# A fused attention and feed-forward kernel: the low parts of the hidden rows move from VectorE to GpSimd

## The reference

```python
def _moe_ref(x, w_gate, w_val, w_out, rms_g):
    rms = np.sqrt(np.mean(x * x, axis=-1, keepdims=True) + 1e-06)
    xn = x / rms * rms_g
    g = xn @ w_gate
    silu = g * (1.0 / (1.0 + np.exp(-g)))
    val = xn @ w_val
    return (silu * val @ w_out).astype(np.float32)
```

## Time and profile before

| | us |
|---|---|
| median of 3 runs | 306.15 |
| lowest, highest | 305.89, 306.91 |
| the profiled execution, its own time | 306.57 |
| its span, first to last instruction | 304.3 |
| TensorE busy in the span | 291.7 |
| VectorE busy | 223.0 |
| ScalarE busy | 165.7 |
| GpSimd busy | 29.8 |

### The profile page before, as it was taken

The page is one execution under the profiler, slowest core; times in us unless marked ns, Lnnn a source line. Parts: engine busy times, 40 slices in busy tenths (PEclk is TensorE's granted clock), DMA queues, the critical chain, the costliest instruction groups (busy, mean ns, idle before and its releaser), DMA issues.

```text
span 304.3 us, 6596 instructions
## 1 busy us (share of the span) xinstructions
PE 291.7 (96%) x2595; PEld 238.0 (78%) x2595; DVE 223.0 (73%) x428; ACT 165.7 (54%) x314; POOL 29.8 (10%) x50
## 2 busy tenths in 40 slices
PE   7789999999999999999999999999999999999983
PEld 7677788888888887888888878887888778797572
DVE  4746977976887879768877797688678767975414
ACT  2565665645656556446565564465546556557422
POOL 1266001000100010003400100020010000000000
PEclk9999999999999999999999999999999999999997
DMA  7999400000013000100130001999300100010007
GB/s 191 324 223 221 101 2 1 2 0 2 0 17 72 19 0 13 28 0 2 16 87 4 0 15 24 380 373 312 68 10 0 26 11 0 13 24 2 2 4 293
DMA packets 34928, 21.94 MB, mean 72 GB/s; under 512 B 19537, under 2 KB 31570, under 8 KB 34898
## 3 DMA queue, kind: packets, MB, share of 16 engines
q1 hardware_dynamic: 34610, 21.23, 26.0%
q10 hardware_dynamic: 288, 0.30, 0.4%
HBM read 17.45 MB, written 2.23 MB: 65 GB/s over the span
## 4 chain that ended last, share of the span: by engine, by line
PE 85%; DVE 4%; DMA 4%; SPq 2%; ACT 2%; issue 2%; DVEq 0%; ACTq 0%
PE bank L956 81%; DMA area<-in_moe_w_out 4%; PE bank L995 2%; PE bank L1029 1%; DVE hl L813 1%; SPq L341 1%; DVE area L948 1%; DVE hid L807 1%; ACT woh L594 1%; DVE area L725 0%; PE bank L1107 0%; DVE cmax_a L864 0%; DVE area L699 0%; PE bank L1042 0%; SPq L347 0%
## 5 line engine op out<-in xcount | busy, mean ns | idle before, releaser
L807 DVE TENSOR_TENSOR hid<-bank,silu 128x512 f32<-128x512 f32 (+1 forms) x108 | 71.0, 658 | 48.2 <-PE bank L956 25.9
L545 ACT ACTIVATE silu<-bank 128x512 f32<-128x512 f32 (+1 forms) x108 | 62.0, 574 | 67.2 <-PE bank L956 66.3
L813 DVE TENSOR_TENSOR hl<-hid,hh 128x512 fp32r<-128x512 f32 (+1 forms) x108 | 71.1, 658 | 0.0
L553 ACT ACTIVATE hh<-hid 128x512 fp32r<-128x512 f32 (+1 forms) x108 | 65.0, 602 | 4.3 <-DVE hid L807 4.3
L956 PE MATMUL bank<-xh,wgh 128*128 128x512 f32 (+1 forms) x108 | 42.9, 397 | 1.8 <-DVE xl L776 1.3
L956 PE MATMUL bank<-hh,woh 128*128 128x512 f32 (+1 forms) x108 | 43.5, 402 | 0.0
L956 PE MATMUL bank<-xh,wvh 128*128 128x512 f32 (+1 forms) x108 | 41.1, 380 | 0.0
L956 PE MATMUL bank<-xh,wvl 128*128 128x512 f32 (+1 forms) x108 | 41.1, 380 | 0.0
L956 PE MATMUL bank<-hh,wol 128*128 128x512 f32 (+1 forms) x108 | 41.1, 380 | 0.0
L956 PE MATMUL bank<-xh,wgl 128*128 128x512 f32 (+1 forms) x108 | 41.0, 380 | 0.0
L956 PE MATMUL bank<-hl,woh 128*128 128x512 f32 (+1 forms) x108 | 40.9, 378 | 0.0
(11 more groups left out here) (147 smaller groups left out, 345.7 us busy)
## 6 DMA issues: line engine op xcount, KB each, us to landing
area<-in_moe_w SPq DMA_DIRECT2D x1, 4096.0 KB, 13.6
area<-in_moe_w SPq DMA_DIRECT2D x8, 512.0 KB, 7.2
q_in<-in_q SPq DMA_DIRECT2D x16, 128.0 KB, 2.8
y_nat<-in_v SPq DMA_DIRECT2D x4, 512.0 KB, 7.1
out<-area SPq DMA_DIRECT2D x8, 256.0 KB, 2.2
area<-in_k SPq DMA_DIRECT2D x14, 128.0 KB, 5.9
y_nat<-area SPq DMA_DIRECT2D x112, 16.0 KB, 1.8
area<-in_moe_w_gate SPq DMA_DIRECT2D x1, 768.0 KB, 7.0
```

The source lines that it names most:

```text
L545: act.activation(silu[n][:, 0:w], gate_b[n][:, 0:w], ACT.Silu).then_inc(s_silu_ready, 1)
L553: act.activation(hh[m % NH][:, 0:w], hid[m % 2][:, 0:w], ACT.Copy).then_inc(s_hh_ready, 1)
L807: dve.tensor_tensor(hid[n][:, 0:w], val_b[n][:, 0:w], silu[n][:, 0:w], ALU.mult).then_inc(s_hid_ready, 1)
L813: dve.tensor_tensor(hl[m % NH][:, 0:w], hid[m % 2][:, 0:w], hh[m % NH][:, 0:w].bitcast(F32), ALU.subtract).then_inc(s_hl_ready, 1)
```

## The change

In `step` of VectorE the low part is left out for the chunks counted 12 to 95 over all blocks, which are all 84 chunks of blocks 1 to 7; those of block 0 and of the narrow block 8 stay. GpSimd makes them instead (`hidden_lo`), in one list with the inverse roots and the row subtractions: the low part of chunk c + 2 in iteration c, the inverse root behind that of iteration 5, the row subtraction behind that of iteration 9. As the first iterations that it covers are 10 and 11 of block 0, each block has its own twelve spread over two iterations of the block before and ten of its own. Two waits join the two engines' turns, one at each end (`s_hl_ready` at C and at C * NB). The constants for the third stage are made in block 0, ahead of the first inverse root of the loop. VectorE's maximum `cmax_a` gets a wait for the copy of the logits, `s_logit_ready`.

```diff
--- before.py
+++ after.py
@@ -320,6 +320,10 @@
 
             return j + 2 <= NB
 
+        def by_pool(i):
+
+            return C <= i < C * NB
+
         def keys_in(j):
 
             return j // 2 + 1 if j % 2 == 0 and j // 2 + 1 < B else 0
@@ -454,25 +458,38 @@
                                    r_blk[:, j, 0:nt].unsqueeze(2).to_broadcast([P, nt, NS]), ALU.subtract)\
                     .then_inc(s_cshift_ready, 1)
 
-            inverse_rms(1)
-            for j in range(2, NB):
-                inverse_rms(j)
-                combine_shift(j - 2)
-                if j == 4:
-                    pool.memset(slotZ[:, :], 0.0)
-                    pool.memset(hTz[:, :, :, :], 0.0).then_inc(done, 1)
-                    pool.memset(ones[:, :], 1.0).then_inc(done, 1)
-                    for n in range(-3, 4):
-
-                        pool.wait_ge(done, 9 + n)
-                        pool.affine_select(out=rep[:, :], in_=rep[:, :], compare_op=ALU.not_equal, fill=1.0, base=NS * n,
-                                           pattern=[[-1, P]], channel_multiplier=1).then_inc(done, 1)
-                if j == 6:
-                    pool.wait_ge(s_vaug_ready, B)
-                    pool.memset(y_nat[:, :, P], 1.0).then_inc(done, 1)
-                    pool.memset(comb[:, NT:NTP, :], 0.0).then_inc(done, 1)
-            inverse_rms(NB)
-            for j in (NB - 2, NB - 1, NB):
+
+            pool.memset(slotZ[:, :], 0.0)
+            pool.memset(hTz[:, :, :, :], 0.0).then_inc(done, 1)
+            pool.memset(ones[:, :], 1.0).then_inc(done, 1)
+            for n in range(-3, 4):
+
+                pool.wait_ge(done, 9 + n)
+                pool.affine_select(out=rep[:, :], in_=rep[:, :], compare_op=ALU.not_equal, fill=1.0, base=NS * n,
+                                   pattern=[[-1, P]], channel_multiplier=1).then_inc(done, 1)
+
+            def hidden_lo(i):
+                m = i % C
+                pool.wait_ge(s_hh_ready, i + 1)
+                pool.tensor_tensor(hl[m % NH][:, :], hid[m % 2][:, :], hh[m % NH][:, :].bitcast(F32), ALU.subtract)\
+                    .then_inc(s_hl_ready, 1)
+
+            for j in range(NB):
+                for c in range(C):
+                    i = C * j + c + LAG - 1
+                    if i == C:
+                        pool.wait_ge(s_hl_ready, C)
+                    if by_pool(i):
+                        hidden_lo(i)
+                    if c == 5:
+                        inverse_rms(j + 1)
+                    if c == 9 and j > 0:
+                        combine_shift(j - 1)
+                    if c == 10 and j == 5:
+                        pool.wait_ge(s_vaug_ready, B)
+                        pool.memset(y_nat[:, :, P], 1.0).then_inc(done, 1)
+                        pool.memset(comb[:, NT:NTP, :], 0.0).then_inc(done, 1)
+            for j in (NB - 1, NB):
                 combine_shift(j)
 
 
@@ -809,6 +826,10 @@
                 jm = j if m < C else j + 1
                 if m >= 0 and (m < C or j < NB):
                     w, i = width(jm), C * j + m
+                    if by_pool(i):
+                        return
+                    if i == C * NB:
+                        dve.wait_ge(s_hl_ready, C * NB)
                     dve.wait_ge(s_hh_ready, i + 1)
                     dve.tensor_tensor(hl[m % NH][:, 0:w], hid[m % 2][:, 0:w], hh[m % NH][:, 0:w].bitcast(F32),
                                           ALU.subtract).then_inc(s_hl_ready, 1)
@@ -861,6 +882,7 @@
                         logits(j - 1)
                     if j == NB - 1 and c == 9:
 
+                        dve.wait_ge(s_logit_ready, NB - 1)
                         dve.tensor_reduce(cmax_a[:, :], logit[:, 0:NC, :].rearrange("p t s -> p s t"), axis=AX.X, op=ALU.max)
                     if last and c == 2:
```

## The result

The changed kernel takes 307.74 us (median of 20 runs, 307.01 to 310.6), the kernel before 305.58 (median of 20, 304.8 to 307.13). The ratio is 1.007, 95% interval 1.0054 to 1.0086: slower by 2.2 us. Forecast were 308.15 us and +2.0.

What follows compares the result with a forecast made beforehand. TensorE was taken to bound the kernel, busy throughout 36 to 257 us. 306.57 + 2.3 - 0.3 = 308.6, 0.4 over the median, so 308.15 us, 0.65% slower; case range 307.3 to 309.0, 8-in-10 range 305.6 to 309.4.

Steps and rivals of the forecast that it cites:

- TensorE can't gain in blocks 1 to 6: From 36 to 257 us TensorE is busy for all of 221.00 us, so taking low parts from VectorE shortens nothing there.
- The low parts on GpSimd have room: GpSimd takes 1.28 us for each low part; late ones cost 0, covered by 1.4 us more of room.
- GpSimd first, then x_n held until it ends, plus 0.55: Blocks 1 to 6: GpSimd starts chunk 8's low part 0.10 us earlier; normalised rows x_n end 0.55 us after it.
- VectorE first: Rival: VectorE starts x_n before GpSimd's low part, so x_n is not held; 305.85 us, no change; chance 0.32.
- The mean is not held: Blocks 1 to 6: the mean square on VectorE ends at its usual length despite GpSimd's low part of chunk 7.
- the mean is held too: Rival, blocks 1 to 6: mean square waits for GpSimd's chunk 7 low part; 0.58 us a block, 309.35 us; chance 0.12.
- the term of +2.3 us: Late x_n makes TensorE lose 0.38 us in each of blocks 1 to 6: 6 x 0.38 = +2.3 us.
- 0.17 us of a late load are absorbed: TensorE weight loads: from block 0's feature transposes, 0.51 us late costs 0.34, so 0.17 is absorbed.
- VectorE is busy for 58 us less: Profile after, whole kernel: VectorE busy for about 58 us less, GpSimd for 108 us more.
- step 2 of the layout: Block 3: the low part behind chunk 8's `hid` goes, which held VectorE's queue for 0.60 us; the mean ends at 137.36.
- Block 7 loses nothing, its end gains 0.3: Block 7: half-wide x_n is ready before its load, no loss; at the end -0.3 us, ends 0 and -0.5.

Runs made afterwards that it cites:

- wait experiment: Changed kernel, but GpSimd waits for the normalised rows x_n before chunk 8's low part in blocks 1 to 7: 304.89 us, ratio 0.9976 to the kernel before.
- memset experiment: Kernel before, with two memsets of 128 x 1024 on GpSimd ahead of the inverse root in blocks 1 to 6: 306.1 us, ratio 0.9999.
- chunk 7 experiment: Changed kernel, with chunk 7's low part, ahead of the inverse root, back on VectorE: 309.4 us, ratio 1.0128 to the kernel before.
- dummy experiment: Kernel before, with an unused 128 x 512 subtraction on GpSimd right behind the inverse root in blocks 1 to 6: 310.82 us, ratio 1.0167.
- with the copy: Kernel before, with an unused 128 x 512 copy on GpSimd behind the inverse root in blocks 1 to 6: 306.94 us, ratio 1.0035.
- constants only: Kernel before, with only the constants for the third stage moved to block 0: 306.14 us, ratio 1.0014.
- chunk 8 on VectorE: Changed kernel, with chunk 8's low part of blocks 1 to 7 back on VectorE, 77 of 84 staying on GpSimd: 304.68 us, ratio 0.9965.

## Why the prediction was right

The direction, the place and the mechanism were right. That 307.74 us lies only 0.4 under the forecast is in part luck (below). Step by step:

- *TensorE can't gain in blocks 1 to 6.* Right. Even with x_n free and 77 low parts off VectorE, the landmarks are 178.20 us apart, against 178.19.
- *The low parts on GpSimd have room.* Right: 1.31 us each for 1.28. In the wait experiment the `hid` of chunk 10 comes 1.1 us later without loss; 1.4 were reckoned as room.
- *GpSimd first, then x_n held until it ends, plus 0.55.* Right in every one of six blocks; VectorE first did not happen. 0.10 us of lead were forecast, 0.07 measured.
- *The mean is not held.* **Wrong, and the reason why the loss in a block was mis-sized.** The rival "the mean is held too" is what the rows show. Its price for a block was 0.58 us, measured are 0.54, since the inverse root came 0.15 us late and not 0.20. So the term of +2.3 us should have been +3.2, and +3.21 is what the landmarks show. The argument against it came from L807, an instruction with a PSUM operand, which says nothing of one that works from SBUF to SBUF. The sentence of the Trainium skill ("SBUF — State Buffer", section "Who interferes with whom", on `tensor_scalar` and GpSimd) was the better guide, and the memset experiment agrees with it: 0.56 us against 0.17.
- *0.17 us of a late load are absorbed.* Right for loads 0.3 to 1.1 us late, with 0.15 to 0.17 absorbed: 0.71 late cost 0.54, in the chunk 7 experiment 0.95 on average cost 0.80, in the dummy experiment 1.06 cost 0.90, with the copy 0.33 cost 0.18.
- *VectorE is busy for 58 us less.* Wrong, 38: the 0.60 us by which a low part holds the queue, used in step 2 of the layout, was not used here, and a wait inside an instruction counts as busy.
- *Block 7 loses nothing, its end gains 0.3.* Right. The load of the narrow block's transposes comes 11.76 us after iteration 2 of block 7, before and after, although the mean (0.68 us) and x_n (1.38 us) are held there too. Rows of the end of block 7 and of block 8 stand below. From iteration 2 of block 7 to the first combine transposes, the kernel takes 31.30 us before (244.88 to 276.18) and 30.91 after (247.85 to 278.76): -0.39.

VectorE in blocks 7 and 8 and the load that waits for it, after:

```profile
263.46 0.42 DVE L824 TENSOR_TENSOR hid<-bank,silu 128x256 f32<-128x256 f32 x1 [1.05 <-POOL hl L474]
263.80 0.70 DVE L804 STREAM_TRANSPOSE area<-yT 128x512 f32<-128x512 f32 x1
264.43 1.78 DVE L886 TENSOR_REDUCE cmax_a<-logit 128x32 f32<-128x896 f32 x1
266.12 0.42 DVE L824 TENSOR_TENSOR hid<-bank,silu 128x256 f32<-128x256 f32 x1
...
266.60 0.19 PEld L978 LDWEIGHTS bank<-xh,wgh 128*128 128x128 f32 x1 [0.54 <-DVE hid L824]
```

The narrow `hid` waits for GpSimd, as laid out, the maximum starts 0.97 us after it, where it was 1.70, and the load's idle time is 0.54 us for 0.92.

With +3.2 and -0.4 the change should cost 2.8 us; the medians say 2.2. Of the 0.6 that are missing, 0.5 lie outside the span: 2.3 us were around it before, 1.8 are now. By spans the change costs 2.6 us (a median of 305.95, against 305.58 - 2.28 = 303.30, reckoned from the time). The two profiled executions differ by less, 1.9 us of span. There 0.24 us are missing before block 1, and 0.7 behind the combine transposes, in 128 small matmuls of the expert stage. TensorE before:

```profile
289.06 3.03 PE L956 MATMUL bank<-area,hTz 128*32 128x128 f32 x101
292.43 1.06 PE L956 MATMUL bank<-area,hTz 128*32 128x128 f32 x27 [0.34 <-issue]
293.43 0.33 PE L1107 MATMUL bank<-ident,comb 128*128 128x128 f32 x1
```

and after:

```profile
291.65 3.70 PE L978 MATMUL bank<-area,hTz 128*32 128x128 f32 x128
295.28 0.33 PE L1129 MATMUL bank<-ident,comb 128*128 128x128 f32 x1
```

4.37 us against 3.63, with a stop of 0.34 before that no engine explains. Other kernels of this study show 3.63 (constants only, chunk 8 on VectorE), 4.37 (the wait for x_n) and 4.1 (the subtraction and the memset behind the inverse root). It goes with no edit that was made. The profiled execution of the kernel before has a span of 304.3 us, where the medians of its spans are 303.45 to 303.6 on three chips, so the 0.7 us are more likely of that execution than of the change; what makes them was not tested.

So the forecast came out near with the help of luck. The held mean that was left out (0.9 us too little) was more than made up by things that were not expected: 0.5 us less around the span, a starting point of three runs that lay 0.6 above the median of twenty (306.15 against 305.58), and 0.3 in small terms. The rest is the 0.4 us by which the forecast lies too high.

## What to carry to other kernels

Work moved off a busy engine changes nothing while another one sets the pace; what it can change is the neighbours of the few short steps on which that one depends. The 84 low parts took no time by themselves here; a few of them took 3.2 us by where they stood. Before an idle engine gets work, list its urgent instructions, here one inverse root of 1.01 us in a block, look at what will stand directly ahead of and behind each, and let the filler wait until the urgent result has been used. And when VectorE and GpSimd meet in SBUF, look at the kind of each instruction (two operands in SBUF, `tensor_scalar` from SBUF to SBUF), since a busy time that trebles looks like work but is a wait. Small differences between kernels are safer to read between two landmarks of a trace than from the times: here half a microsecond of time moved outside the span.

## What was not expected of the hardware

- A mean over 4 columns, 0.17 us of work, waits until a GpSimd instruction has ended (0.51 us beside a subtraction), and also for one that only writes (0.56 us beside a memset); a product of two SBUF operands does not mind that memset (0.70) but waits for a GpSimd copy (1.08) or subtraction (1.78).
- Not every GpSimd instruction that reads holds for its length. A low part on VectorE lay inside the inverse root, a power on 4 columns that lasts from 138.04 to 139.05, and took its usual 0.68 us, by the timeline of VectorE in block 3 of the kernel before:

```profile
138.51 0.68 DVE L813 TENSOR_TENSOR hl<-hid,hh 128x512 fp32r<-128x512 f32 x1
```

- The seven selects of the constants took 0.37 us more in block 0, where two low parts of VectorE lie inside their stretch, than in block 3, where one does; the low parts kept their time. That the low parts are what stretches them was not tested.
- The race for x_n was won by GpSimd, whose next instruction follows the inverse root on the same engine, while x_n is released by a semaphore. It started 0.06 to 0.11 us ahead in all 30 cases: six blocks each in the changed kernel, the chunk 7 run, and the runs with a subtraction, a copy and a memset behind the inverse root.
